# Products and output parts of the last stage share a ring of eight PSUM banks; two of four token sums move to the middle of a pair

## What is computed

```python
# attention, 4 x 8 heads, 576 tokens, head size 64
scores = where(s >= max(s) - tau, s, -1e9);  attn = softmax(scores);  x = attn @ v
# first layer pair, 2304 tokens, 512 -> 2048 -> 512
h = x @ w_in;  y = (max(h, 0) + alpha * min(h, 0)) @ w_out
# second, 512 -> 1024 -> 512
out = (((y @ w1) * (y @ w2)) @ w3) @ w_out2
```

## Time and profile before

| | |
|---|---|
| median of 3 runs | 1061.4 us (1058.37 to 1063.78) |
| profiled execution | 1063.7 us, span 1061.9 |
| mean granted TensorE clock | 0.971 of full |
| busy | PE 980.5, DVE 671.2, POOL 513.2, ACT 416.8 us |
| stage before the last | about 541.8 to 752.6 us |
| last stage | 752.6 us to the end |
| matmuls in these two | L771 768, L785 768 (second half), L820 1344, L832 768 |

### The profile page before, as it was taken

The page is one execution under the profiler, slowest core; times in us unless marked ns, Lnnn a source line. Parts: engine busy times, 40 slices in busy tenths (PEclk is TensorE's granted clock), DMA queues, the critical chain, the costliest instruction groups (busy, mean ns, idle before and its releaser), DMA issues.

```text
span 1061.9 us, 18253 instructions
## 1 busy us (share of the span) xinstructions
PE 980.5 (92%) x6656; PEld 882.8 (83%) x6656; DVE 671.2 (63%) x1646; ACT 416.8 (39%) x976; POOL 513.2 (48%) x604
## 2 busy tenths in 40 slices
PE   3789967999999999999989999999998998998998
PEld 2566644787777787879989999999998998998998
DVE  6878878999999898922332434344747547546543
ACT  5656656666666656534323233323212102102110
POOL 4867758766665666423433333333516225215222
PEclk9799986999999999999999999999999999998999
DMA  7379899687878677767153222221500200200001
GB/s 260 81 218 276 247 283 257 180 240 188 217 210 223 182 208 196 180 179 286 54 206 120 90 90 96 97 102 65 223 4 12 79 1 17 73 1 23 24 1 45
DMA packets 57017, 146.95 MB, mean 138 GB/s; under 512 B 8544, under 2 KB 24928, under 8 KB 54880
## 3 DMA queue, kind: packets, MB, share of 16 engines
q1 hardware_dynamic: 45936, 113.35, 35.2%
q10 hardware_dynamic: 10992, 32.45, 11.0%
HBM read 74.33 MB, written 27.79 MB: 96 GB/s over the span
## 4 chain that ended last, share of the span: by engine, by line
PE 53%; DVE 17%; DMA 7%; issue 6%; SPq 6%; POOL 6%; ACT 4%; ACTq 1%; POOLq 0%; DVEq 0%
PE psum L820 17%; PE psum L785 11%; PE psum L832 9%; PE psum L771 8%; DVE nmx L1085 5%; DMA zbuf<-ybuf 4%; SPq L517 4%; PE psum L730 4%; DVE e_ring L1098 4%; PE psum L692 2%; POOL g L1296 2%; PE psum L743 2%; DVE g_raw L1130 2%; PE psum L675 1%; DMA raw_a<-weights 1%
## 5 line engine op out<-in xcount | busy, mean ns | idle before, releaser
L1296 POOL TENSOR_TENSOR g<-g_raw,g 128x288 fp32r<-128x288 f32 x160 | 131.5, 833 | 230.4 <-ACT g L961 214.0
L675 PE MATMUL psum<-ks,qs 128*128 128x288 f32 x640 | 122.5, 322 | 37.8 <-DVE e_ring L1098 24.9
L1325 POOL TENSOR_SCALAR e_ring<-e_ring,rden,uni 128x576 f32<-128x576 f32 x144 | 118.6, 824 | 62.1 <-DVE rden L1109 58.8
L675 PEld LDWEIGHTS psum<-ks,qs 128*128 128x128 f32 x640 | 102.2, 206 | 54.5 <-DVE e_ring L1098 35.5
L922 ACT ACTIVATE e_ring<-psum,nmx 128x576 f32<-128x576 f32 x144 | 106.7, 741 | 84.9 <-DVE nmx L1085 84.7
L1130 DVE SCALAR_TENSOR_TENSOR g_raw<-g_raw,beta_sb,psum 128x288 f32<-128x288 f32 x128 | 65.2, 512 | 100.0 <-ACT g_raw L957 99.4
L832 PE MATMUL psum<-g,w_b 128*128 128x288 f32 x768 | 115.8, 308 | 13.1 <-DVE y_buf L1191 10.1
L832 PEld LDWEIGHTS psum<-g,w_b 128*128 128x128 f32 x768 | 108.3, 197 | 19.7 <-DVE y_buf L1191 12.5
L1085 DVE TENSOR_REDUCE nmx<-psum 128x1 f32<-128x576 f32 x144 | 108.4, 753 | 25.9 <-PE psum L675 25.5
L1098 DVE SCALAR_TENSOR_TENSOR e_ring<-psum,thr,e_ring 128x576 f32<-128x576 f32 x144 | 115.3, 800 | 12.2 <-ACT e_ring L922 11.7
L692 PE MATMUL psum<-zbuf,vs 128*64 128x320 f32 (+1 forms) x640 | 109.0, 435 | 12.7 <-DMA zbuf<-ybuf 9.5
(11 more groups left out here) (81 smaller groups left out, 1416.9 us busy)
## 6 DMA issues: line engine op xcount, KB each, us to landing
zbuf<-ybuf SPq DMA_DIRECT2D x96, 180.0 KB, 4.6
zbuf<-ybuf SPq DMA_DIRECT2D x96, 144.0 KB, 4.3
xy<-xs SPq DMA_DIRECT2D x12, 1152.0 KB, 5.2
raw_a<-weights SPq DMA_DIRECT2D x49, 256.0 KB, 7.0
q_raw<-q ACTq DMA_DIRECT2D x16, 576.0 KB, 6.3
xs<-x_hl SPq DMA_DIRECT2D x32, 288.0 KB, 6.1
k_raw<-k ACTq DMA_DIRECT2D x15, 576.0 KB, 7.4
zbuf<-ybuf ACTq DMA_DIRECT2D x32, 180.0 KB, 4.9
```

The source lines that it names most:

```text
L675: last = mm(dst, qs[:, par, at:at + P], ks[:, par, part, h, cols], start=(m == 0), stop=(m == 2 * len(terms) - 1))
L1296: sub = lambda out_, a, hi: nc.gpsimd.tensor_tensor(out_, a, hi.bitcast(F32), ALU.subtract)
L1325: nc.gpsimd.tensor_scalar(e, e, rden[:, i:i + 1], uni[:, i:i + 1], ALU.mult, ALU.add)\
```

## The change

Products and output parts of a half pair now take their banks in one order: 28 products and 8 parts are 36 turns (`HALF_DUO`), turn modulo 8 is the bank, and `bank_free` waits for whatever read the bank eight turns earlier. The fourth held buffer is a slot of `spare` for both parities, and VectorE waits for GpSimd's product of the block before (`s_c`) before it is written. Of the token sums of the next pair, T3 goes to a buffer of its own (`t3_raw`) and T1 over the token part (1, 0) in `y_in`, both behind the second evacuation of the pair's first half; T2 and T4 stay at the pair's end. In the stage before, `weight_sums` stands behind f=5 instead of f=1, five of the seven splits stand at other places, and the weight pieces are loaded before SyncE's wait for the last stores.

```diff
--- before.py
+++ after.py
@@ -83,7 +83,6 @@
 
 
 SEVEN = 7
-SEVEN_BANKS = 6
 A11, S2, A12, S1, S3, S4, A22 = range(SEVEN)
 X11, T2, X21, T1, T3, X22, T4 = range(SEVEN)
 DUOS = NCH // 2
@@ -95,7 +94,9 @@
 READ = [0, 1, 2, 5, 4, 6, 7]
 PARTS = 2 * KD
 
-S_SPLIT = {(0, 3): 0, (0, 5): 1, (0, 7): 2, (1, 1): 3, (1, 3): 4, (1, 5): 5, (1, 7): 6}
+HALF_DUO = SEVEN * FT // 2 + PARTS
+
+S_SPLIT = {(0, 7): 0, (1, 0): 1, (1, 1): 2, (1, 2): 3, (1, 4): 4, (1, 5): 5, (1, 7): 6}
 
 EARLY = N_WP + N_M1
 Q_STEPS = {2: 0, 4: 1}
@@ -284,7 +285,7 @@
             y_in = sb("y_in", [2, KD, CH], F32, place)
         xy = [sb("xy_0", [2, KD, CH], F32R), None]
         g = sb("g", [2, FT, CH], F32R)
-        g_raw = sb("g_raw", [RAW + 1, CH])
+        g_raw = sb("g_raw", [RAW, CH])
 
         warm = sb("warm", [2], F32, attn)
         share = sb("share", [1], F32, attn)
@@ -316,6 +317,7 @@
             spare = sb("spare", [2 * KD, CH], F32, place)
         xy[1] = sb("xy_1", [2, KD, CH], F32R)
         y_buf = sb("y_buf", [KD, CH])
+        t3_raw = sb("t3_raw", [2, CH])
 
         psum = ctx.enter_context(nc.psum_tensor("psum", [P, 8, 512], F32))
 
@@ -481,18 +483,25 @@
             return y_in[:, c, 2 * kh:2 * kh + 2, :]
 
         def token_source(k):
-            at = {X11: (0, 0), X21: (0, 1), X22: (1, 1)}
-            return y_part(*at[k]) if k in at else token_sum(k)
+
+            at = {X11: (0, 0), X21: (0, 1), X22: (1, 1), T1: (1, 0)}
+            return y_part(*at[k]) if k in at else t3_raw[:, :, :] if k == T3 else token_sum(k)
+
+        def product_turn(at, k):
+            return HALF_DUO * (at // (FT // 2)) + SEVEN * (at % (FT // 2)) + k
+
+        def part_turn(n):
+            return HALF_DUO * (n // PARTS) + SEVEN * FT // 2 + n % PARTS
 
         def seven_bank(at, k):
-            return psum[:, (SEVEN * at + k) % SEVEN_BANKS, 0:CH]
+            return psum[:, product_turn(at, k) % 8, 0:CH]
 
         def held(at, i):
 
-            return (spare if at % 2 else g_raw)[:, i, :]
-
-        def part_bank(i):
-            return psum[:, 6 + i % 2, 0:CH]
+            return (spare if at % 2 or i == RAW else g_raw)[:, i, :]
+
+        def part_bank(n):
+            return psum[:, part_turn(n) % 8, 0:CH]
 
         def out_part(i):
 
@@ -602,10 +611,11 @@
                 load_chunk(xs, c, c)
                 sp.wait_ge(s_ye, KD * (ck + 1))
                 sp.dma_start(yp[ck], y_buf[:, :, :]).then_inc(s_yp_out, 16)
-            sp.wait_ge(s_yp_out, 16 * 2 + 16)
             for q in range(GROUPS):
                 for i, x in enumerate((A11, S1, A12, A22)):
                     sp.dma_start(weights_of(q, x, True)[:, 1, :], weights[EARLY + N_M1 + 4 * q + i]).then_inc(s_s_in[q], 16)
+
+            sp.wait_ge(s_yp_out, 16 * 2 + 16)
 
             def load_duo(p):
                 sp.dma_start(y_in[:, :, :, :], ys[2 * p:2 * p + 2].rearrange("c p k t -> p c k t")).then_inc(s_duo_in, 16)
@@ -801,20 +811,26 @@
                 hidden(NCH + ck, w_b, 0, ck % 2, 16 * (ck // 2) + 32)
                 down_half(NCH + ck, w_b, SLOTS // 2)
 
+            def bank_free(turn):
+
+                half, i = divmod(turn - 8, HALF_DUO)
+                if turn < 8:
+                    if turn >= 4:
+                        pe.wait_ge(s_ye, (2 * NCH - 1) * KD + (turn - 4) + 1)
+                elif i >= SEVEN * FT // 2:
+                    pe.wait_ge(s_oe, PARTS * half + i - SEVEN * FT // 2 + 1)
+                elif i % SEVEN == A11:
+                    pe.wait_ge(s_p1, FT // 2 * half + i // SEVEN + 1)
+                else:
+                    pe.wait_ge(s_sum, SUMS * (FT // 2 * half + i // SEVEN) + READ[i % SEVEN])
+
             def one_of_seven(at, k):
 
                 p, m = divmod(at, FT)
                 if m == 0:
                     for by in range(2):
                         pe.wait_ge(s_tl[by], seven_counts(p, k + 1)[by])
-                if SEVEN * at + k >= SEVEN_BANKS:
-                    old, x = divmod(SEVEN * at + k - SEVEN_BANKS, SEVEN)
-                    if x == A11:
-                        pe.wait_ge(s_p1, old + 1)
-                    else:
-                        pe.wait_ge(s_sum, SUMS * old + READ[x])
-                elif k >= 4:
-                    pe.wait_ge(s_ye, (2 * NCH - 1) * KD + (k - 4) + 1)
+                bank_free(product_turn(at, k))
                 for j in range(2):
                     for wp, xp in ((0, 0), (0, 1), (1, 0)):
                         last = mm(seven_bank(at, k), weights_of(2 * (m // 4) + j, k)[:, wp, (m % 4) * P:(m % 4 + 1) * P],
@@ -824,12 +840,12 @@
             def out_terms(p, h, i, fs):
 
                 n, c = PARTS * (2 * p + h) + i, 1 - i // KD
-                if 0 in fs and n >= 2:
-                    pe.wait_ge(s_oe, n - 1)
+                if 0 in fs:
+                    bank_free(part_turn(n))
                 for f in fs:
                     pe.wait_ge(s_cl, 2 * (FT * p + h * FT // 2 + f) + 2 - c)
                     for wp, gp in ((0, 0), (0, 1), (1, 0)):
-                        last = mm(part_bank(i), w_b[:, wp, SLOTS // 2 + h * FT // 2 + f, i % KD * P:(i % KD + 1) * P],
+                        last = mm(part_bank(n), w_b[:, wp, SLOTS // 2 + h * FT // 2 + f, i % KD * P:(i % KD + 1) * P],
                                   g[:, gp, 2 * f + c, :], start=(f + wp + gp == 0), stop=(f == FT // 2 - 1 and wp == 1))
                 if FT // 2 - 1 in fs:
                     last.then_inc(s_o, 1)
@@ -842,7 +858,6 @@
                         one_of_seven(FT * p + m, k)
                     if m % 4 == 3:
                         if p == 0:
-                            pe.wait_ge(s_ye, 2 * NCH * KD)
                             pe.wait_ge(s_wc_in[m // 4], 16)
                         for i in range(0, PARTS, 2):
                             for fs in (range(FT // 2 - 1), [FT // 2 - 1]):
@@ -1028,7 +1043,7 @@
                     act.wait_ge(s_p, SEVEN * (FT * p - 1) + k + 1)
                 act.wait_ge(s_duo_in, 16 * (p + 1))
                 if k in (T1, T2, T3, T4):
-                    act.wait_ge(s_ts, 4 * p + {T1: 1, T2: 2, T3: 3, T4: 4}[k])
+                    act.wait_ge(s_ts, 4 * p + {T3: 1, T1: 2, T2: 3, T4: 4}[k])
                 copy(tokens_of(k)[:, 0, :, :], token_source(k)).then_inc(s_th, 1)
 
             def first_product(at):
@@ -1205,17 +1220,20 @@
                 dve.wait_ge(s_sh, SEVEN * q + k + 1)
                 sub(weights_of(q, k)[:, 1, :], weights_of(q, k, True)[:, 1, :], weights_of(q, k)[:, 0, :]).then_inc(s_sl[1], 1)
 
-            def token_sums(p):
+            def early_token_sums(p):
+                dve.wait_ge(s_duo_in, 16 * (p + 1))
+                less(t3_raw[:, :, :], y_part(1, 1), y_part(1, 0)).then_inc(s_ts, 1)
+                less(y_part(1, 0), y_part(1, 0), y_part(0, 0)).then_inc(s_ts, 1)
+
+            def late_token_sums(p):
+
                 if p == 0:
                     dve.wait_ge(s_h, 2 * NCH * FT)
                 else:
                     dve.wait_ge(s_p, SEVEN * FT * p)
-                dve.wait_ge(s_duo_in, 16 * (p + 1))
-                less(token_sum(T1), y_part(1, 0), y_part(0, 0)).then_inc(s_ts, 1)
-                dve.wait_ge(s_ts, 4 * p + 1)
-                less(token_sum(T2), y_part(1, 1), token_sum(T1)).then_inc(s_ts, 1)
-                less(token_sum(T3), y_part(1, 1), y_part(1, 0)).then_inc(s_ts, 1)
                 dve.wait_ge(s_ts, 4 * p + 2)
+                less(token_sum(T2), y_part(1, 1), y_part(1, 0)).then_inc(s_ts, 1)
+                dve.wait_ge(s_ts, 4 * p + 3)
                 less(token_sum(T4), y_part(0, 1), token_sum(T2)).then_inc(s_ts, 1)
 
             def token_operand_lo(p, k):
@@ -1239,6 +1257,8 @@
                 dve.wait_ge(s_p, SEVEN * at + S3 + 1)
                 add(held_1, bank(S3), held_1).then_inc(s_sum, 1)
                 dve.wait_ge(s_sum, SUMS * at + 4)
+                if at >= 1:
+                    dve.wait_ge(s_c, at)
                 add(held_3, bank(S1), held_1).then_inc(s_sum, 1)
                 dve.wait_ge(s_p, SEVEN * at + S4 + 1)
                 add(held_2, bank(S4), held_2).then_inc(s_sum, 1)
@@ -1251,21 +1271,22 @@
                 n = PARTS * (2 * p + h) + i
                 dve.wait_ge(s_o, n + 1)
                 if h == 0:
-                    nc.vector.tensor_copy(out_part(i), part_bank(i)).then_inc(s_oe, 1)
+                    nc.vector.tensor_copy(out_part(i), part_bank(n)).then_inc(s_oe, 1)
                 else:
                     dve.wait_ge(s_oe, n - PARTS + 1)
-                    add(out_part(i), part_bank(i), out_part(i)).then_inc(s_oe, 1)
+                    add(out_part(i), part_bank(n), out_part(i)).then_inc(s_oe, 1)
 
             for ck in range(NCH):
                 for f in range(FT):
                     activation_of(NCH + ck, f, 1, psum[:, f % 4, 0:CH])
-                    if (ck % 2, f) == (0, 1):
+                    if (ck % 2, f) == (0, 5):
                         weight_sums(ck // 2)
```

(7 more changed lines are left out.)

## The result

| | before | after |
|---|---|---|
| median | 1061.18 us (1058.37 to 1063.78, 4 runs) | 1036.24 us (1031.63 to 1037.64, 4 runs) |
| profiled execution | 1063.7 us, span 1061.9 | 1037.64 us, span 1035.7 |

The ratio is 0.9758, with a 95% interval from 0.9717 to 0.9799: 24.9 us, or 2.4%, faster. The forecast was 1036.

What follows compares the result with a forecast made beforehand. TensorE, busy 92%, was taken as the bound, with 25.2 us excess in the last stage; 9.8 (banks) + 15.4 (token sums) + 0.3 (weight part) = 25.5 us gain, 1036 us from median 1061.4, range 1031 to 1046.

Steps and rivals of the forecast that it cites:

- the excess of 25.2 us: Last stage: time the four pairs take beyond 70.34 us each without waits; all of it was expected to go.
- My 6 to 7 us of slack: Pair end: operand 0 ready near 816.9, wanted at 824.2, so operands for the next pair's first products are not late.
- the banks: Last stage: one eight-bank ring removes the parts' waits for evacuations, the small excess in eight half pairs; gain 9.8 us.
- the token sums: Three pair ends: two sums instead of four before the first evacuation; the 15.4 us there come back whole.
- The weight part: Stage before: weight sums at f=5, later splits, earlier loads; net gain 0.3 us, bounds +4.5 and -6.6.
- Both signs: Even chunks of the stage before: first gains 3.19 us, three others lose 0.95 each, -2.85 together.
- The new waits: Waits added by the eight-bank ring and shared fourth buffer; taken to cost 0 us.
- (B): Pair boundary keeps part of its stall because VectorE and GpSimd operands or evacuations come late; some 9 us kept, 1045; chance 0.12.
- (C): Stage before: f=5 stalls bring the clock down or are twice the figure; 1043; chance 0.11.
- (D): Slower: shared `held_3` makes VectorE wait in each of 31 blocks; 1067 or more; chance 0.02.
- (E): Short gaps between groups drop the clock: 1051, chance 0.03, or whole last stage slow, about 1190, chance 0.01.
- (F): Waits do not do what they say, e.g. a part still waits for its predecessor; 1061; chance 0.01.

Runs made afterwards that it cites:

- experiment 7: Kernel before with the eight-bank ring alone, plus 2, 4, 8 extra sums ahead of the four token sums of pairs 1, 2, 3: 1050.65 us.
- experiment 8: Kernel of experiment 4 with the two late token sums of a pair's end moved behind the first evacuation: 1029.73 us.
- Experiment 1: Kernel before with only the eight-bank ring for products and parts; token sums, weight sums and splits as before: 1037.8 us.
- experiment 2: Changed kernel with six product banks, two part banks, weight sums, splits and load order as before; moved token sums and shared fourth buffer kept: 1047.17 us.
- experiment 5: Changed kernel with the weight sums back at f=1, new splits and early loads kept: 1034.45 us.
- experiment 9: Kernel before with the ring, weight sums at f=3, new splits, early loads, and all four token sums behind the first evacuation of a pair's end: 1029.38 us.
- experiment 4: Changed kernel with the weight sums behind f=3 instead of f=5: 1029.66 us.

## Why the prediction was right

**The bound, the excess of 25.2 us.** Right: the last stage lost 24.8. The two floors came out as taken, 22.39 us for a run and 12.72 for eight parts where I had 12.80. The 0.4 us between 25.2 and 24.8 is mostly the three pair ends, which stay 0.2 over 12.80. VectorE's timeline of the changed kernel, first in the middle of pair 0, then at its end:

```profile
777.24 0.75 DVE L1207 TENSOR_TENSOR t_raw<-y_in 128x576 f32<-128x576 f32 x1
...
809.65 0.75 DVE L1207 TENSOR_TENSOR raw_b<-y_in 128x576 f32<-128x576 f32 x1
810.43 1.25 DVE L1207 TENSOR_TENSOR raw_b<-y_in,raw_b 128x576 f32<-128x576 f32 x1
811.82 0.46 DVE L1206 TENSOR_TENSOR y_buf<-psum,y_buf 128x288 f32<-128x288 f32 x1
```

The two moved sums (the second, at 777.90, takes the same) take 0.75 us each in VectorE's idle time, at the lower end of the bound (at most 2.7 for both). At the end two sums stand before the first evacuation at 811.82, and the first low part takes 0.77, the two others 1.62 and 1.43. GpSimd's low parts of the fourth block, in the middle of the pair and at its end, and the last of its operands:

```profile
774.81 1.58 POOL L1319 TENSOR_TENSOR g<-spare,g 128x288 fp32r<-128x288 f32 x2 [0.54 <-ACT g L1063]
...
809.92 2.43 POOL L1319 TENSOR_TENSOR g<-spare,g 128x288 fp32r<-128x288 f32 x2 [0.55 <-ACT g L1063]
...
818.03 1.42 POOL L1319 TENSOR_TENSOR w_b<-raw_b,w_b 128x576 fp32r<-128x576 f32 x1
```

It ends at 818.03 + 1.42 = 819.45; TensorE wants that operand at 821.74 + 4.8 = 826.5, 7.1 us later. My 6 to 7 us of slack were right for the operands. I did not work out the evacuations of parts 1 to 3, which stand behind the low parts and whose banks products 1 to 3 take; experiment 7 shows that these end last when VectorE is late. What I took as zero and isn't: the two low parts take 2.43 us at the pair's end against 1.58 in the middle, and the fourth block's terms wait for them, 13.00 us for the parts instead of 12.72. 0.28 x 3 = 0.8 us; experiment 8 removes it.

**The division of the 25.2 was wrong as an attribution.** The prediction booked 9.8 us to the banks and 15.4 to the token sums. Experiment 1 shows 25.1 for the banks alone: with eight banks no part waits for an evacuation, so the sums at the pair's end may take 5 us and hide behind the 12.8 us of parts. I used that very argument for the operands (slack of 6 us) and did not apply it to four sums instead of two. The total stood, since with both edits made it does not matter which of them is credited.

**The weight part.** Both signs within the part as foreseen, the gain of the first chunk and the loss of the others; the net came out with the other sign. Stall 1.57 us where I had 1.33, so three chunks lose 1.2 each, not 0.95, and the first gains 2.95, not 3.19: 0.6 us lost instead of 0.3 gained. The duration of the four sums (3.75 from 550.34 to 554.09 in the chain, 3.76 taken from the earlier trace rows) was right, and so was the end of the wait: the last low part lets TensorE go on at 556.66, 4.12 us after the end of L781 (539.74 + 12.80), and I had 4.13. Inside these 4.12 us there are two waits, 0.97 for low part 6 and about 0.35 for low part 7, with three matmuls between. What is missing is the restart: the 75 matmuls behind the wait take 10.25 us, not 75/96 of 12.80 = 10.00. 1.32 + 0.25 = 1.57. The same shows behind other waits at full clock: 24 matmuls take 3.43 us instead of 3.20 behind 0.15 in experiment 2, the first chunk of experiment 5 is 0.25 longer than its wait of 0.72 explains, and the 0.18 in experiment 7 cost 0.41. What TensorE does in that time no run shows. The 0.38 of before hides the same quarter, since the 75 matmuls there take 10.26. By the exclusion that the Trainium skill states (SBUF — State Buffer, Who interferes with whom) the four sums could have taken 4.4 us and the gain been 23; they took 3.75.

**The new waits.** Zero, as taken, to about 0.2 us in the whole stage: the profile shows no wait of TensorE on the ring. In experiment 9, which has no shared fourth buffer and no sums in the middle of a pair, the second run of products in each pair takes 22.33 us, in the changed kernel 22.39, together 0.24 us; which of the two edits costs it was not tried.

**The rivals.** (B) is excluded by 70.50 us a pair, and experiment 7 says what it would have needed: some 4 us more of VectorE's work. (C): waits of 0.97 and 0.35 us brought no slower clock, and the stall was 1.57 where twice my figure would be 2.66. (D) and (E): no such wait, clock 1.00. (F): the last stage got 24.8 us shorter, so the waits do what they say. The size in microseconds, 1036 against 1036.24, is closer than the method deserves, and in part luck. By the stages of the two traces the change is worth 24.8 - 0.6 = 24.2 us, 1.3 less than the 25.5 of the forecast; and the part that the change does not touch moved by 2.0 us between the two profiles, about as much as the 2.3 us that the forecast took off for the distance of the profiled execution to its median.

## What to carry to other kernels

When a consumer has two banks of its own beside a ring of six for the producer, put both in one ring: the wait for an evacuation is put off by six more turns, and work that stands in front of the evacuation on its engine is hidden, here up to 5 us of sums and some 4 us more, not without end. Two edits that remove the same stall do not add up; make each alone before crediting it. In these traces a wait of TensorE cost its length and about 0.25 us behind it. Work put in front of an engine's time-critical chain should be early enough that the queue behind it catches up before the deadline: moved from f=5 to f=3, the same 3.75 us cost 0.1 us instead of 1.57.

## What was not expected of the hardware

Two gaps of 1.12 and 0.85 us, with six matmuls between them, were followed by the lower clock: in experiment 7 the granted clock was 0.85 and 0.83 in the stretches from 970.0 to 980.6, with TensorE busy 3.62 of the first 5.6 us; the six matmuls from 973.86 took 1.73 us where 0.97 is usual. In steps of 2 us it was 1.00, 0.98, 0.50, 0.67 and again 1.00 from 978 on: the lower of the two levels, 1.2 GHz, stood for some 3 us. Waits of 0.97 and 0.35 us amid dense work, in the changed kernel, left it at 1.00. This is one execution, and the two cases differ in more than the length of the gaps.

The time before 540 us, whose instructions are the same in all kernels, is where the runs differ: the stage with L781 began at 539.74 us in the changed kernel, at 537.18 in experiment 4, at 545.95 in experiment 1 and at 547.6 in experiment 7. Behind that point the same code took the same time to 0.1 us, but for stretches in which the lower clock was granted: the three pair ends of before took 18.74, 19.18 and 19.49 us. So stages were compared by their length in the trace, and times only by medians. Why the first stages differ by up to 10 us was not tried.
